# An attention tile's vector work moved about one step earlier inside a fused attention and MLP kernel

## The reference, cut to what matters

```
mask = np.abs(pos[:, None] - pos[None, :]) < factor      # factor = 4
scores = np.where(mask, scale * q @ k.T, -1e9)
out_local = softmax(scores) @ v
x = (out_up + out_local)                                  # 2304 x 512
rms = np.sqrt(np.mean(x * x, axis=-1, keepdims=True) + 1e-06)
xn = x / rms * rms_g
h = silu(xn @ w_gate) * (xn @ w_val)                      # 512 -> 1536
y = h @ w_out                                             # 1536 -> 512
r = np.maximum(y @ w_in, 0.0)                             # 512 -> 2048
out = (s * r * r + b) @ w_out2                            # 2048 -> 512
```

## Time and profile before

| what | value |
|---|---|
| median of three runs | 1020.36 us |
| the profiled execution's own time | 1020.36 us |
| its span on the core | 1017.2 us |
| PE busy | 958.8 us (94%) |
| DVE busy | 528.0 us (52%) |
| POOL busy | 414.8 us (41%) |
| ACT busy | 330.2 us (32%) |

### The profile page before, as it was taken

The page is one execution under the profiler, slowest core; times in us unless marked ns, Lnnn a source line. Parts: engine busy times, 40 slices in busy tenths (PEclk is TensorE's granted clock), DMA queues, the critical chain, the costliest instruction groups (busy, mean ns, idle before and its releaser), DMA issues.

```text
span 1017.2 us, 12760 instructions
## 1 busy us (share of the span) xinstructions
PE 958.8 (94%) x4836; PEld 766.6 (75%) x4864; DVE 528.0 (52%) x785; ACT 330.2 (32%) x706; POOL 414.8 (41%) x216
## 2 busy tenths in 40 slices
PE   4398899998999999999999999999999999999997
PEld 3276688975777767777777898887888888888896
DVE  4568777876765676555542223334433343333343
ACT  2244564334312431243133344223222232222232
POOL 4788889887786577555620255100000000000000
PEclk9999999999999999999999999999999999999999
DMA  9986346421422132101103232101101100100010
GB/s 256 284 249 192 98 127 185 145 85 55 140 63 63 55 104 75 41 28 62 37 1 124 94 120 99 42 1 42 42 0 37 47 1 1 63 1 1 0 43 21
DMA packets 54376, 79.38 MB, mean 78 GB/s; under 512 B 9836, under 2 KB 37068, under 8 KB 52908
## 3 DMA queue, kind: packets, MB, share of 16 engines
q1 hardware_dynamic: 53212, 73.86, 24.4%
q10 hardware_dynamic: 1104, 4.72, 1.2%
HBM read 67.05 MB, written 11.50 MB: 77 GB/s over the span
## 4 chain that ended last, share of the span: by engine, by line
PE 76%; POOL 7%; DVE 7%; issue 3%; ACT 2%; DMA 2%; SPq 1%; ACTq 0%; POOLq 0%; DVEq 0%
PE bank L726 22%; PE bank L848 6%; PE bank L849 6%; PE bank L850 6%; PE bank L866 6%; PE bank L867 6%; PE bank L868 6%; PE bank L762 4%; PE bank L760 4%; PE bank L761 4%; POOL prod L531 3%; POOL prod L545 2%; DMA rawk<-in_k_dram 2%; PE bank L1475 1%; DVE sc L551 1%
## 5 line engine op out<-in xcount | busy, mean ns | idle before, releaser
L531 POOL TENSOR_TENSOR prod<-qs,ks 128x896 f32<-128x896 f32 x80 | 177.0, 2236 | 69.6 <-DVE sc L551 57.3
L545 POOL TENSOR_TENSOR prod<-sc,vs 128x896 f32<-128x896 f32 x80 | 150.4, 1988 | 60.9 <-DVE x L561 40.1
L887 DVE SCALAR_TENSOR_TENSOR r<-bank,r 128x512 f32<-128x512 f32 (+1 forms) x80 | 51.1, 638 | 183.7 <-ACT r L875 183.7
L850 PE MATMUL bank<-y_h,w2i_l 128*128 128x512 f32 (+1 forms) x320 | 117.7, 368 | 0.0
L782 DVE TENSOR_TENSOR bank<-bank,u 128x512 f32<-128x512 f32 (+1 forms) x66 | 39.5, 599 | 125.5 <-PE bank L726 120.2
L875 ACT ACTIVATE r<-bank 128x512 f32<-128x512 f32 (+1 forms) x80 | 44.4, 555 | 183.7 <-PE bank L850 183.0
L760 PE MATMUL bank<-h_h,wo_h 128*128 128x512 f32 (+1 forms) x264 | 102.7, 389 | 0.0
L551 DVE TENSOR_REDUCE sc<-prod 128x14 f32<-128x896 f32 x80 | 85.3, 1078 | 32.4 <-POOL prod L531 32.4
L726 PE MATMUL bank<-x_h,wv_h 128*128 128x512 f32 (+1 forms) x264 | 100.4, 392 | 0.0
L561 DVE TENSOR_REDUCE x<-prod 128x128 f32<-128x896 f32 x80 | 85.8, 1079 | 17.4 <-POOL prod L545 17.1
L762 PE MATMUL bank<-h_h,wo_l 128*128 128x512 f32 (+1 forms) x264 | 93.2, 353 | 0.0
(11 more groups left out here) (131 smaller groups left out, 1911.6 us busy)
## 6 DMA issues: line engine op xcount, KB each, us to landing
raww<-in_moe_w_out_dram SPq DMA_DIRECT2D x14, 512.0 KB, 3.7
ks<-in_k_dram SPq DMA_DIRECT2D x16, 280.0 KB
vs<-in_v_dram SPq DMA_DIRECT2D x16, 280.0 KB, 5.1
y_scr<-y_st ACTq DMA_DIRECT2D x4, 1024.0 KB, 3.8
raww<-in_moe_w_in_dram SPq DMA_DIRECT2D x8, 512.0 KB, 4.0
y_raw<-y_scr SPq DMA_DIRECT2D x4, 1024.0 KB, 4.8
out_dram<-o_st SPq DMA_DIRECT2D x16, 256.0 KB, 2.8
rawq<-in_q_dram SPq DMA_DIRECT2D x3, 1152.0 KB, 12.3
```

Source lines behind the costliest of these rows:

```text
L531: pool.tensor_tensor(dst, qv, kv, ALU.mult).then_inc(prod_ready, 1)
L545: pool.tensor_tensor(dst, pv, vv, ALU.mult).then_inc(prod_ready, 1)
L850: last = pe.matmul(o, w2i_l[:, m, kk, :], y_h[t % 2][:, kk, 0:w], start=False, stop=kk == DT - 1)
```

## The change

Five tables are replaced. In them the reductions of tile 1 stand earlier (QK1_AT, PV1_AT), pieces 12 to 17 of the weights are copied one step earlier (HI_AT), piece 16's low part is formed in step 12 and not 13 (LO_AT), and on POOL piece 13 moves behind product pv 7 (from pv 6), piece 15 behind pv 11 (from pv 15). On DVE softmax_max goes from step 6 to 5, softmax_norm from 7 to 6, the first add_pooled from step 12 (ahead of the reductions) to 11 (behind them), the second from 14 to 13, inverse_root_of from 15 to 14. On ACT the exponential goes from step 7 to 6, the first squares from 13 to 12, the second squares from step 15, behind silu(15), to step 13, behind hidden_hi(13), and normalise from one block of four in step 16 to two pairs in step 15, before and behind hidden_hi(15).

```diff
-HI_AT = {0: (6, 7), 2: (8,), 4: (9,), 5: (10,), 6: (11,), 8: (12,), 9: (13,), 10: (14,), 12: (15,), 13: (16,), 14: (17,)}
-LO_AT = {0: (4,), 2: (6,), 4: (8,), 7: (10,), 9: (12,), 11: (14,), 13: (16,)}
-QK1_AT = {0: (7, 8), 1: (9,), 3: (10, 11), 4: (12,), 5: (13, 14), 6: (15,)}
-PV1_AT = {8: (0, 1), 9: (2, 3), 10: (4, 5), 11: (6, 7), 12: (8, 9, 10), 13: (11, 12), 14: (13, 14, 15)}
-
-REST_AT = {("qk", 7): (5,), ("qk", 10): (7,), ("qk", 15): (9,), ("pv", 3): (11,), ("pv", 6): (13,), ("pv", 15): (15, 17)}
+HI_AT = {0: (6, 7), 2: (8,), 4: (9,), 5: (10,), 6: (11,), 7: (12,), 9: (13, 14), 11: (15,), 12: (16,), 13: (17,)}
+LO_AT = {0: (4,), 2: (6,), 4: (8,), 7: (10,), 9: (12,), 11: (14,), 12: (16,)}
+QK1_AT = {0: (7, 8), 1: (9, 10), 3: (11, 12), 4: (13,), 5: (14, 15)}
+PV1_AT = {7: (0,), 8: (1, 2), 9: (3, 4), 10: (5, 6), 11: (7, 8), 12: (9, 10, 11, 12), 13: (13, 14, 15)}
+
+REST_AT = {("qk", 7): (5,), ("qk", 10): (7,), ("qk", 15): (9,), ("pv", 3): (11,), ("pv", 7): (13,), ("pv", 11): (15,), ("pv", 15): (17,)}
...
-                if s == 7:
+                if s == 6:
                     softmax_exp(act, 1)
-                if s == 13:
+                if s == 12:
                     squares(act, 1, 0)
                 if s == 15:
-                    squares(act, 1, 1)
-                if s == 16:
-                    normalise(act, range(FAC), 2)
+                    normalise(act, (0, 1), 2)
...
                 hidden_hi(act, s)
+                if s == 13:
+                    squares(act, 1, 1)
+                if s == 15:
+                    normalise(act, (2, 3), 2)
...
+                    if s == 5:
+                        softmax_max(dve, 1)
                     if s == 6:
-                        softmax_max(dve, 1)
-                    if s == 7:
                         softmax_norm(dve, 1)
                         qk_reduce(dve, 2, 0)
                         qk_reduce(dve, 2, 1)
-                    if s == 12:
-                        add_pooled(dve, 1, 0)
                     for n in PV1_AT.get(s, ()):
                         pv_reduce(dve, 1, n)
+                    if s == 11:
+                        add_pooled(dve, 1, 0)
+                    if s == 13:
+                        add_pooled(dve, 1, 1)
                     if s == 14:
-                        add_pooled(dve, 1, 1)
-                    if s == 15:
                         inverse_root_of(dve, 1)
```

## The result

The changed kernel took 1033.04 us (median of four runs, 1032.11 to 1034.49) against 1020.78 us before, a ratio of 1.0124 with a 95% interval of 1.0101 to 1.0145: 12 us slower, where 1032.3 was forecast. The profiled execution took 1034.91 us, with a span of 1032.8 us. Two single executions in what follows, one of the query-key half alone (1367.57 us at a granted clock of 0.69) and one of the kernel before (1577.59 us), are left out of the medians and ratios.

The account below looks back on a forecast made before the run. PE was taken as the bound, with one 4.8 us stall for tile 1's x. That stall goes, but gate(15) comes late, so the transposes start 11.9 us later, clock 0: 1020.36 + 11.9 = 1032.3 us, range 1023 to 1038.

Parts of the forecast that it names:

- The mechanism: Steps 12 to 14: late POOL products delay DVE's add_pooled, then ACT's squares, then silu(14); gate(15) at 237.1, not 220.45.
- the largest term: Step 13: second squares, behind pv 15 and second add_pooled on DVE, stand ahead of silu(14); PE stands 12 us at gate(15).
- Steps 1 to 3: Reducing qk 10 in step 1 starts hidden_mul(2) and PE's next transposes 2.0 us later; a later stall swallows it.
- POOL gets ahead by 0: POOL's gain from its own waits taken as 0, other end 5.1 us; product pv 8 ready at 210.0.
- The clock nets to 0: Lower clock moves with the stall from gate(17) to gate(15): 1.7 us lost there, 1.7 us not lost here.
- The sum: Tile 1's transposes start at 253.65, not 241.76: +11.9 us, giving 1032.3 us.
- The rule on POOL and DVE: DVE with two SBUF inputs or two-port mode and POOL reading SBUF exclude each other; second add_pooled costs 1.57 us at most.
- the stall simply goes: First rival, chance 0.06: x ready at PE's arrival, no silu late; -4.76 - 1.7 gives 1013.9 us.
- The bound of 1021.8: Rival, chance 0.06: DVE never keeps POOL waiting; gate(15) still 6.1 us late, 1021.8 us, no change.
- The last rival: Chance 0.10: long stall costs more than itself, by lower clock, slower products or late value windows; 1036 to 1042.

Follow-up runs that it names:

- the query-key half alone: Kernel before, with only QK1_AT, softmax_max, the exponential and softmax_norm as in the change, value half as before: 1022.35 us, ratio 1.0021.
- the query-key half undone: Changed kernel, with QK1_AT, softmax_max, the exponential and softmax_norm as before, value half of the change kept: 1030.15 us, ratio 1.0117.
- The hold on POOL: Kernel before, with one more wait on POOL: tile 2's first product after tile 1's pv 15 waits for tile 1's 1/rms: 1019.87 us, ratio 0.9992.
- the kernel with five reductions in step 16: Kernel before, with The hold on POOL, 1/rms ahead of hidden_lo(15), two x slices scaled by DVE, tile 2's qk 2 and 3 moved to step 16: 1024.05 us, ratio 1.0044.

## Why the prediction was right, step by step

**The mechanism** that holds gate(15) was right in each link, and the largest term is shown: take the squares from ahead of silu(14), and 8.1 of the 17.6 us by which gate(15) was late behind step 0 (92.8 against 75.2; 16.7 were forecast) are gone at once, with nothing else changed. What the copies and low parts of the weights cost by themselves was tried for piece 15 alone.

**Places**, with 1.21 us taken off: gate(14) at 218.4 (forecast 216.8), hidden_mul(13) at 227.1 (225.8), gate(15) at 238.0 (237.1), tile 1's transposes at 256.7 (253.65). The wait at gate(14) was 2.76 us (2.7). That at gate(15) was 9.59 and not 12, though gate(15) itself was 0.9 later than forecast: PE ended step 14 at 228.4 and not 225.1, half because gate(14) came 1.6 later, half because step 14, run partly at the lower clock, took 10.0 us and not 8.3. A wait is shorter when PE is late; the start is the safer thing to forecast.

**Steps 1 to 3** were mis-sized. The transposes did start 2 us late (the wait was 2.50 instead of 0.59), but the lower clock behind that wait cost some 1.5 us more: the transposes and the 12 matmuls of out1 took 3.4 us (165.44 to 168.88) and before 1.9 (162.30 to 164.20). So it is 3.5 us. That the term vanishes in the long wait holds only roughly in the changed kernel (undone, it gives back 1.4 us at gate(15) and 0.9 of the tile stretch), and hardly at all where that long wait is missing (3.2 of 3.5 remain).

**POOL gets ahead by 0**: it did not get ahead, but fell behind. pv 0 did start 1.2 us sooner behind step 0, and POOL then waited 2.09 us ahead of pv 2. DVE had pv 8 at 211.4 (with the 1.21 off), where 210.0 was forecast. With the query-key half undone it had it at the forecast place, 64.8 us behind step 0, so it is the delay of step 3 that reaches POOL, through reductions that stand behind hidden_mul. These 1.4 us, less what the second add_pooled saved, are roughly the 0.9 us by which gate(15) missed its place.

**The clock nets to 0** was wrong. Two stretches behind the new waits ran at 0.61 and 0.52, where the earlier trace rows had one at 0.68. Columns are length, busy (instructions) of PE, PEld, DVE, ACT, POOL, granted clock, DMA share and GB/s:

```profile
219.60:224.00 4.40, 4.40 (x13) 2.75 (x14) 3.43 (x4) 0.00 (x0) 2.70 (x2) 0.61 0.00 0
239.20:244.20 5.00, 4.75 (x12) 3.13 (x13) 4.30 (x4) 0.60 (x1) 5.00 (x3) 0.52 0.00 0
```

The first lies in the shadow of gate(15). The second stretched the way from gate(15) to the transposes to 18.7 us (16.55 forecast), 2.2 us; and step 17, which was to give 1.7 back, took 10.9 us instead of 11.5, as a wait of 0.81 us for x_l appeared in it; the remaining 0.3 us are not traced. So 1.6 us and not 0, in this execution: by the later wait of 2.4 us, another one might have kept the full clock at one of these places.

**The sum** by the traces is 0.9 for gate(15) and 1.6 for the clock above the forecast 11.9, 14.4 us in the profiled execution, which was itself 1.9 us above its median. The medians differ by 12.3 us. That the median came within a microsecond of the forecast is partly luck: by stretch the forecast was 2.5 us short, and the starts of step 0 alone spread by 4 us between traces.

**The rule on POOL and DVE** (the Trainium skill, SBUF — State Buffer, section Who interferes with whom) held. With POOL waiting for piece 17's copy, the second add_pooled took 1.23 us, under the 1.57 assumed and well under the 2.19 of the earlier trace rows; with piece 15 put back beside it, it took 2.14. The hold on POOL shows the same for the short instructions of 1/rms.

**The rivals.** That the stall simply goes did not happen, though x was ready: in the changed kernel the last slices were scaled at 250.4, 7.5 us ahead of PE. The bound of 1021.8 for a POOL that is never kept waiting was not reached. DVE's 4.46 us of 4.8, counted there for the first rival as slack, are 93% busy. The last rival's late value windows appeared once: POOL waited 0.80 us for one ahead of pv 10 (215.25), which cost nothing, since DVE reduced pv 10 only behind 220.14. The gain that was found is 4.5 us, and it took three edits together: the hold, which makes the 1/rms chain short, its place ahead of hidden_lo(15), and the later reductions. The hold alone and the other two alone gained nothing.

## What to carry to other kernels

On an engine that runs in order, ask of each instruction that is moved not only when its result is ready, but what stands behind it if it waits: four squares of 2 us held PE for 8 us, because they stood ahead of a silu. Before work is moved ahead of a stall, look at the lengths on the chain that ends it: a small instruction that takes ten times its usual length and ends when another engine's does may be worth more than a new order. And a reordering that wins at one wait is often repaid at the next one down the chain (the hold alone won 2.8 us at the transposes and gave 2.6 back before step 18), so both must be opened together.

## What the runs showed of the hardware

- Small DVE instructions on 128 x 4 numbers, among them a tensor_scalar with one SBUF input, end only when POOL's running product ends (1.97 and 2.05 us beside 0.16), and with POOL waiting they take 0.15 to 0.17. A larger one, add_pooled with two SBUF inputs, took 1.23 us with POOL idle and 2.14 beside a weight piece. Two 128x512 tensor_scalars took 4.66 us beside two products; their length with POOL idle was not measured.
- The lower clock is not a matter of the wait's length alone. Behind one and the same wait of 2.42 to 2.44 us, near 575 us in the kernel before, it was 1.00 over 5 us in six traces and 0.66 to 0.70 in seven, at a price of some 1.6 us. At gate(14), in the 4.40 us behind a wait of 2.76 us the granted clock was 0.61 (the changed kernel), and in the 4.98 us behind one of 3.37 us it was 1.00 (the same with the query-key half undone). In 5 us behind a wait of 2.00 us at the same transposes the granted clock was 0.66 (the hold alone), behind one of 3.33 us it was 1.00 (the kernel with five reductions in step 16). What else decides it was not tried. (A granted clock of 1.00 is 2.4 GHz, 0.50 is 1.2 GHz.)
- The start of step 0 varied by 4 us from one execution to the next, and PE's longest wait ahead of it, which ends near 45 us and is for DVE's pooled q of the second batch, goes with a part: 14.7, 15.8 and 16.8 us in the traces where step 0 began at 142.40, 145.22 and 146.43. A difference of a few microseconds between two traces in one of these kernels has to be looked for there first.
